# A lead of 224 bytes in place of 192 ahead of the buffers that stream through TensorE

## The reference

```python
qn = q / (norm(q, axis=1) + 1e-06); kn = k / (norm(k, axis=1) + 1e-06)
s = kn.transpose(0, 2, 1) @ qn / tau          # 256 x 256, contracted over 6016 tokens
a = softmax(s)
x = v @ a
h = x @ w_in1;  x = (h * cos(h)) @ w_out1      # first MLP
h = x @ w_in2;  y = (h * sigmoid(h)) @ w_out2  # second MLP
```

## Time and profile before

| | |
|---|---|
| three runs | 1072.27, 1074.94 and 1080.47 us; median 1074.94 |
| the profiled execution | 1074.97 us, span 1073.0 us |
| TensorE matmul busy | 1050.5 us, 98% of the span, 8718 records |
| VectorE busy | 954.5 us, 89% |
| ScalarE busy | 804.9 us, 75% |
| mean share of the 2.4 GHz clock granted | 0.995 |

### The profile page before, as it was taken

How to read it: one execution, slowest core, us unless ns; L and a number is a source line. 1 busy time by engine, 2 the same in 40 slices (tenths; PEclk the granted TensorE clock), 3 DMA queues, 4 the chain that set the end, 5 groups by cost and what they waited for, 6 DMA issues and landing times. The chain is left out here.

```text
span 1073.0 us, 21180 instructions
## 1 busy us (share of the span) xinstructions
PE 1050.5 (98%) x8718; PEld 1043.9 (97%) x8718; DVE 954.5 (89%) x1061; ACT 804.9 (75%) x875; POOL 0.8 (0%) x7
## 2 busy tenths in 40 slices
PE   7989999999999999999999999999999999999997
PEld 7979999999999999999998899999999999999997
DVE  7999989999999999998887389999999999999987
ACT  7778777778787778787676477886787787777775
POOL 0000000000000000000000000000000000000000
PEclk9999999999999999999999899999999999999999
DMA  8820011230330321304137201001101101101000
GB/s 282 293 77 21 1 55 32 98 129 2 128 128 2 129 74 56 129 20 159 37 136 311 92 21 36 25 16 40 41 2 41 40 2 40 40 2 40 21 21 20
DMA packets 18286, 76.03 MB, mean 71 GB/s; under 512 B 1809, under 2 KB 5905, under 8 KB 16145
## 3 DMA queue, kind: packets, MB, share of 16 engines
q1 hardware_dynamic: 18192, 74.72, 19.8%
HBM read 47.71 MB, written 27.00 MB: 70 GB/s over the span
## 5 line engine op out<-in xcount | busy, mean ns | idle before, releaser
L1230 PE MATMUL banks<-g_lo,w1out 128*128 128x256 f32 (+1 forms) x768 | 215.3, 280 | 0.0
L1231 PE MATMUL banks<-g_hi,w1out 128*128 128x256 f32 (+1 forms) x768 | 215.3, 280 | 0.0
L1229 PE MATMUL banks<-g_hi,w1out 128*128 128x256 f32 (+1 forms) x768 | 215.2, 280 | 0.0
L1229 PE MATMUL banks<-g_hi,o2w 128*128 128x256 f32 (+1 forms) x672 | 189.3, 282 | 3.7 <-DVE g_lo L956 1.6
L1229 PE MATMUL banks<-xf_hi,h1w 128*128 128x256 f32 (+1 forms) x672 | 189.4, 282 | 2.9 <-ACT banks L469 2.0
L1229 PE MATMUL banks<-xf_hi,h2w 128*128 128x256 f32 (+1 forms) x672 | 189.8, 282 | 2.3 <-ACT s_part L477 1.3
L1230 PE MATMUL banks<-xf_lo,h2w 128*128 128x256 f32 (+1 forms) x672 | 189.4, 282 | 0.0
L1231 PE MATMUL banks<-xf_hi,h2w 128*128 128x256 f32 (+1 forms) x672 | 189.4, 282 | 0.0
L1230 PE MATMUL banks<-g_lo,o2w 128*128 128x256 f32 (+1 forms) x672 | 189.1, 281 | 0.0
L1231 PE MATMUL banks<-g_hi,o2w 128*128 128x256 f32 (+1 forms) x672 | 189.1, 281 | 0.0
L1230 PE MATMUL banks<-xf_lo,h1w 128*128 128x256 f32 (+1 forms) x672 | 188.5, 280 | 0.0
(11 more groups left out here) (122 smaller groups left out, 2318.6 us busy)
## 6 DMA issues: line engine op xcount, KB each, us to landing
w_scr<-w_split SPq DMA_DIRECT2D x8, 1792.0 KB, 8.9
qk_raw<-qk SPq DMA_DIRECT2D x23, 512.0 KB, 4.7
h2w<-w_scr SPq DMA_DIRECT2D x4, 1792.0 KB, 8.1
o2w<-w_scr SPq DMA_DIRECT2D x4, 1792.0 KB, 8.5
form<-v_tiles SPq DMA_DIRECT2D x11, 512.0 KB, 4.9
x_scr<-xo SPq DMA_DIRECT2D x11, 512.0 KB, 2.9
form<-x_scr SPq DMA_DIRECT2D x11, 512.0 KB, 4.2
y_tiles<-xo SPq DMA_DIRECT2D x11, 512.0 KB, 5.0
```

The costliest lines, as they stand in the source:

```text
L1229: nc.tensor.matmul(out, w_hi, m_hi, start=start, stop=False, skip_group_check=True)
L1230: nc.tensor.matmul(out, w_hi, m_lo, start=False, stop=False, skip_group_check=True)
L1231: return nc.tensor.matmul(out, w_lo, m_hi, start=False, stop=stop, skip_group_check=True)
```

## The change

`stream_lead` grows from 48 to 56 floats. It is the only edit. Every buffer behind it begins 32 bytes later, so the streaming buffers lie 224 bytes behind a multiple of 512 where they lay 192 behind. The weights keep their places, and so do `qk_hi` and `qk_lo`. Nothing else moves: the order of the instructions on every engine is the same, row by row.

```diff
@@ -111,7 +111,7 @@
-        sb("stream_lead", [P, 48])
+        sb("stream_lead", [P, 56])
         form = sb("form", [P, 8, HALF])
         xf_hi = sb("xf_hi", [P, 2, 7, HALF], F32R)
         xf_lo = sb("xf_lo", [P, 2, 7, HALF], F32R)
```

## The result

| | before | after |
|---|---|---|
| median of 20 runs | 1072.03 us | 1080.67 us |
| lowest to highest | 1058.12 to 1080.48 us (and one of 1726.38) | 1076.91 to 1084.7 us |
| the profiled execution | 1074.97 us, span 1073.0 | 1079.96 us, span 1078.0 |

The change makes the kernel slower: the ratio after to before is 1.014, with a 95% interval of 1.0119 to 1.016. (The ratio is taken over the runs within 1.5% of the fastest of their kernel, which leaves out the upper part of the runs of before; the medians of all 20 are 0.8% apart.) The runs of before are spread over 22 us, those of after over 8. The kernel before, run again in four later groups of 17 to 23 runs, had medians of 1075.2 to 1075.8 us; beside these the changed kernel is 5 us slower, 0.5%. So the sign is sure, and the size lies between 0.5 and 1.4%, by which runs of before one takes.

What follows compares the result with a forecast made beforehand. The pace of TensorE's matmul starts in 830 us of the MLPs was taken as the bound. 1074.97 - 31.7 (113.3 ns pace) + 5.3 (given back to VectorE) = 1048.6 us, range 1034 to 1098 us.

Steps and rivals of the forecast that it cites:

- the sign: Whole kernel: faster, 1048.6 us from 1074.97; chance of faster by over 1% 0.43, within 1% 0.28, slower 0.29.
- What bounds the kernel: Both MLP stretches, 830 us: the pace of TensorE's matmul starts, 117.8 ns each, the only thing the change can act on.
- the excess over the columns: 256-column matmuls in both MLPs: 11.1 ns above 106.7 each, 78 us in all, most likely operand supply, no fixed instruction price.
- the two paces are two locks of the same stream: MLP matmuls: 113.3 ns (641 to 664 us) and 117.8 ns are two lasting patterns, chosen by how data and weight reads coincide.
- One reading behind it: Near 608 us at half clock: starts 213 ns apart, twice 106.7, taken to show the excess gone there.
- The step that failed: Both MLP stretches: the new distance runs at 113.3 ns in place of 117.8, 31.7 us less.
- the chance of faster ahead of slower: Whole kernel: faster 0.43 against slower 0.30, because the present pattern was the worse of two, with a dearer one only inferred.
- The rival "slower": Both MLPs: reads meet where both lose, 2.7 to 3.1 ns more per matmul, 19 to 22 us, 1094 to 1097; chance 0.30.
- The mechanism I gave it: Wide matmuls in both MLPs: every weight load lengthened by 4 ns, not one in three, giving 120.5 ns per matmul.
- The rival "nothing changes": Both MLPs: 117.8 ns is the rest position whatever the addresses; 1075 us, 1068 to 1081; chance 0.27.
- What VectorE would give back: Heavy steps of both MLPs: TensorE would wait for VectorE and at times fall to the slower pace; 5.3 us given back.
- The Trainium skill's rule: SBUF: TensorE has separate read ports for moving operand and weights and waits on no one; the lead would be worth nothing.

Runs made afterwards that it cites:

- bare stream: A kernel of matmuls and weight loads alone, 256 columns, one weight and one data buffer, at many data-to-weight distances: 113.3 to 123.4 ns; at 192 both 113.3 and 117.8.
- silent192: The kernel before (distance 192) cut to TensorE's two MLPs, without waits inside them or other engines' work: 113.3 ns in the first MLP, 117.8 in the second.
- map_busy: Matmuls alone at distances 32, 112, 192, 224, with VectorE, ScalarE, both or neither at work: 116.7, 113.3, 117.8, 118.4 ns in all phases.
- silent kernels: TensorE's two MLPs alone, without waits or other engines' work, at distances 112, 192, 224: 118.7 and 120.0 ns; 113.3 and 117.8; 2538 matmuls in 300 us.
- map16: Matmuls alone at 32 distances, 0 to 496 bytes in steps of 16, four entries each: 256 to 496 repeat the lower ones to 0.1 ns.
- lead448: The kernel before with stream_lead at 112 floats instead of 48, distance 448 instead of 192: median 1074.66 us, ratio 1.0007.

## Why the prediction was wrong

The range of 1034 to 1098 us held the time; the sign did not.

**What bounds the kernel** was right: the pace in the 830 us of the earlier trace rows, nothing else. The difference of 5.0 us between the two executions is 42 matmuls fewer at that pace. That the excess over the columns is not a fixed price, and that the two paces are two locks of the same stream, was right as well: the bare stream has more than ten different paces between 113.3 and 123.4 ns with the same instructions.

One reading behind it was wrong. The earlier trace rows are matmuls of 192 columns, and the prediction set their 213 ns against 256 columns, so these rows do not show that the excess is gone at half clock. The trace after has the wide ones, at a granted clock of 0.50 (592 to 595 us):

```profile
592.22 0.42 PE L1230 MATMUL banks<-g_lo,w1out 128*128 128x256 f32 x1
...
595.00 0.41 PE L1231 MATMUL banks<-g_hi,w1out 128*128 128x256 f32 x1
```

Thirteen starts in 2.78 us are 214 ns each, against 213.3 for 256 columns. The intervals are 213 to 214 ns at the distances 112, 256 and 448 as well, in whose traces such matmuls fell under the half clock too. So the conclusion holds, though the rows that it was drawn from do not show it: the excess, and with it the effect of the distance, is there at 2.4 GHz alone.

**The step that failed** is "I take the faster lock as the value, since it is the one other pace that these buffers and instructions have shown". It took a second lock *of distance 192* for what another distance would give, and so put the term at 31.7 us less, where the pace of 224 made it 5.0 us more. The same step put the chance of faster ahead of slower. Each distance has locks of its own. Why a distance has the ones that it has, no run shows. 224 has only 118.1 to 118.6 ns; it lost 192's 113.3 and got nothing for it. The trace of before could not tell that, as all its 256-column matmuls behind the lead stand at one distance; what the earlier trace rows do say is that 192 has something to lose.

**The rival "slower"** was right in sign, and mis-sized: I charged 2.7 to 3.1 ns per matmul from the excesses of the 384 and 512-column matmuls, and it was 0.55 ns (118.33 - 117.78). (The excess of 14.2 in that sum stands in no row: the earlier trace rows give 14.4 and 13.3.) The mechanism I gave it, a longer weight load in all three passes, is not what happened: the one longer load got shorter, to 188 ns like the others. At distance 256, by contrast, the price of 2.2 ns (120.0) came close to it.

**The rival "nothing changes"** had named a successor 120 ns later at distance 0 in `chunk`. That was no sign of a common rest position: the bare stream at 0 has 120.0.

**What VectorE would give back** was right as a mechanism. The fast stretch ends behind a copy of ScalarE, which is late behind VectorE, in two traces. I had priced it at 5.3 us of waits and short falls into the slower lock; its price is larger, since behind the 10 ns slip the slower lock held for the whole rest of the MLP, 396 us. So before did not use its better lock much.

**The 8.6 us between the medians** are more than the 5.0 between the two profiled executions, and than the 5 us to the later medians of before: this first group of before has 9 of its 20 runs below 1070 us, the later ones one to three of 17 to 23. Two things spread the runs of before. One goes with the granted clock: in one later group the run with a mean of 1.0 took 1071.14 us, one with 0.99 took 1079.88. The other is not the clock: in the same groups single runs took 1065.13, 1067.13 and 1067.96 us at a mean of 0.994, where the others at 0.994 took 1073 to 1077. Such runs may have held 113.3 ns for longer. If one held it through the first MLP as silent192 does, it would save 434 x (1 - 113.33 / 117.78) = 16.4 us and take 1058.6; the fastest took 1058.12. No profile caught such a run, so this is argued and not shown. At 224 there is no such lock, and none of its 20 runs is below 1076.91.

**The Trainium skill's rule** ("SBUF — State Buffer", "Who interferes with whom") stands half confirmed. That TensorE waits on no other engine at the SBUF is what map_busy (VectorE and ScalarE) and the silent kernels beside the whole ones at 112 and 224 (the DMAs too) show to 0.1 ns. That its two reads are independent of each other is not what they show: with the same instructions the distance between the two operands moves the pace from 113.3 to 123.4 ns. The measurement decides.

## What to carry to other kernels

Where a weight load and a matmul of 256 columns follow each other without a gap, read the pace from the starts and compare it with columns / 2.4 GHz. An excess of 7 to 13 ns is worth a sweep of the distance between moving and stationary buffers, in small steps over 256 bytes, with the kernel's own stream of matmuls and no other engine, and then in the whole kernel. That own stream had the whole kernel's pace at 112 and 224 in both MLPs; at 192 it had 113.3 ns in the first, where the profiled whole kernel had 117.8. A bare loop met whole kernels at 32, 224 and 256 bytes to 0.1 ns, but at 112 it misled by 5 to 7 ns, though it showed one pace only there. A pace that can be lost through a wait of 10 ns is no gain to count on. What could be counted on here was a distance at which neighbouring locks cost little: 32 has 116.7 ns nearly always and 117.8 or 117.9 at its worst, which is about the old pace. The gain was 6.6 us, 0.5%.

## What the runs showed of the hardware that was not expected

The pace has a period of 256 bytes in the distance, not 512 (map16; lead448 equal to before). It is sensitive to 4 bytes: 113.3 ns at 112, 122.0 at 116. It locks into patterns that last for thousands of matmuls, some 3840 in silent192, and which one holds can depend on the few matmuls ahead. VectorE's and ScalarE's accesses to SBUF don't touch it (map_busy). At half clock (0.50 granted) the intervals are 213 to 214 ns at 112, 224, 256 and 448 alike. I had expected any of these to be blurred in a kernel with four engines at work; at 112 and 224 the counts in 300 us agree with the silent kernel to a matmul or two.
